# Attention scores turned on VectorE instead of TensorE, with a new start order and finer weight splits, in a fused attention, MLP and mixture-of-experts kernel

## What is computed

```python
scores  = scale * x @ state.T ;  a  = softmax(scores, -1) ;  xread = a @ state     # over Ns = 32
scores2 = scale * state @ x.T ;  a2 = softmax(scores2, -1);  sread = a2 @ x        # over S = 512
x = concat([xread, sread], 2) -> 4608 rows of 512
h = x @ w_in ; g = h * clip(h + 3, 0, 6) / 6 ; x = g @ w_out                       # first MLP
e_idx = argmax(x @ w_gate) ; out = gate * sigmoid(...) * (relu(x @ w1[e]) @ w2[e]) # one expert per row
```

## Time and profile before

| | us |
|---|---|
| median of 3 runs | 1210.06 (1208.73 to 1210.42) |
| the profiled execution | 1208.73 |
| its span, first to last instruction | 1207.0 |
| TensorE busy | 1170.7 (97%) |
| VectorE busy | 602.6 (50%) |
| ScalarE busy | 443.7 (37%) |

### The profile page before, as it was taken

One profiled execution on the slowest core, in us unless ns is written; L12 is line 12 of the kernel. 1 busy time (PEld: TensorE's weight loads), 2 busy tenths in 40 slices (PEclk: granted clock), 3 DMA queues, 4 the chain that ended last, 5 costly groups with the idle time before them and its releaser, 6 DMA issues.

```text
span 1207.0 us, 21126 instructions
## 1 busy us (share of the span) xinstructions
PE 1170.7 (97%) x6652; PEld 923.6 (77%) x6653; DVE 602.6 (50%) x1140; ACT 443.7 (37%) x741; POOL 83.9 (7%) x96
## 2 busy tenths in 40 slices
PE   8999999999999999999999987999999999999995
PEld 6777777777777777777778975888888888878874
DVE  5564644645536456455464355645453333666331
ACT  3454434443444344444544341423331112344110
POOL 0000100101001001010010110200000000000000
PEclk9999999999999999999999988999999999999998
DMA  9210110001101010010020365145151111442111
GB/s 368 71 36 1 71 36 36 36 36 71 35 1 71 36 35 36 36 71 1 1 105 1 122 226 171 54 175 188 33 189 37 52 35 45 179 152 59 46 37 42
DMA packets 46922, 91.45 MB, mean 76 GB/s; under 512 B 10751, under 2 KB 32895, under 8 KB 42496
## 3 DMA queue, kind: packets, MB, share of 16 engines
q1 hardware_dynamic: 41088, 72.57, 17.7%
q0 software_dynamic: 5760, 17.90, 3.9%
HBM read 65.95 MB, written 25.55 MB: 76 GB/s over the span
## 4 chain that ended last, share of the span: by engine, by line
PE 93%; DVE 3%; ACT 1%; issue 1%; DMA 0%; POOL 0%; DVEq 0%; ACTq 0%; SPq 0%; POOLq 0%
PE y_ps L840 31%; PE h_ps L896 17%; PE y_ps L922 17%; PE h_ps L825 14%; PE y_ps L908 3%; PE a_ps L800 2%; PE h_ps L815 2%; PE a_ps L690 1%; PE y_ps L861 1%; PE a_ps L778 1%; PE a_ps L751 1%; PE b_ps L698 1%; DVE we L469 1%; PE b_ps L690 1%; PE b_ps L715 0%
## 5 line engine op out<-in xcount | busy, mean ns | idle before, releaser
L840 PE MATMUL y_ps<-w_out_hi,hid_hi 128*128 128x512 f32 x544 | 220.4, 405 | 0.3 <-DVE w_out_lo L1329 0.3
L840 PE MATMUL y_ps<-w_out_hi,hid_lo 128*128 128x512 f32 x544 | 212.8, 391 | 0.0
L840 PE MATMUL y_ps<-w_out_lo,hid_hi 128*128 128x512 f32 x544 | 212.6, 391 | 0.0
L896 PE MATMUL h_ps<-we,xg_t_hi 128*128 (+1 forms) x608 | 197.4, 406 | 7.1 <-DVE xg_t_lo L1399 3.9
L922 PE MATMUL y_ps<-we,act_t_hi 128*128 (+1 forms) x608 | 187.9, 390 | 1.7 <-issue 1.7
L825 PE MATMUL h_ps<-att_hi,mix 128*128 128x512 f32 x512 | 185.6, 406 | 0.4 <-DVE att_lo L1212 0.4
L1344 DVE SCALAR_TENSOR_TENSOR hid<-hid,h_ps 128x512 f32<-128x512 f32 (+1 forms) x144 | 94.3, 655 | 181.8 <-ACT hid L1037 180.3
L1037 ACT ACTIVATE hid<-h_ps,three 128x512 f32<-128x512 f32 (+1 forms) x144 | 95.5, 663 | 203.1 <-PE h_ps L825 179.7
L840 PEld LDWEIGHTS y_ps<-w_out_hi,hid_hi 128*128 128x128 f32 x544 | 102.2, 188 | 51.2 <-issue 30.4
L896 PEld LDWEIGHTS h_ps<-we,xg_t_hi 128*128 128x128 f32 x608 | 113.6, 192 | 33.2 <-issue 8.4
L922 PEld LDWEIGHTS y_ps<-we,act_t_hi 128*128 128x128 f32 x608 | 114.1, 188 | 26.8 <-issue 2.0
(11 more groups left out here) (226 smaller groups left out, 1324.4 us busy)
## 6 DMA issues: line engine op xcount, KB each, us to landing
raw<-in_w SPq DMA_DIRECT2D x14, 2048.0 KB, 8.4
xg<-buckets SPq DMA_DIRECT2D x164, 64.0 KB
xb<-in_x_rows SPq DMA_DIRECT2D x8, 1024.0 KB, 4.8
x_t<-in_x_t SPq DMA_DIRECT2D x7, 1024.0 KB, 5.0
buckets<-pad_row SPq DMA_DIRECT2D x8, 774.0 KB, 8.7
w_in_raw<-in_w_in SPq DMA_DIRECT2D x4, 1024.0 KB, 13.1
raw_out<-in_w_out SPq DMA_DIRECT2D x4, 1024.0 KB, 14.7
x_t_second<-in_x_t SPq DMA_DIRECT2D x1, 1024.0 KB, 19.9
```

The costliest lines, as they stand in the source:

```text
L840: i = pe.matmul(y_ps[:, t, :], (hid_hi, hid_lo)[hp][:, hid_at(b, j), t * P:(t + 1) * P], w_out_s[wp][:, j, :], start=(j == 0 and m == 0), ...
L896: i = pe.matmul(hid_ps[:, h, :], xg_t[xp][:, slot % 2, k, :], we[:, bass.ds(w_at + (wp * WPART + k * F + h * BANK), BANK)], start=(k == 0 ...
```

## The change

- **Turning.** S1's banks are no longer copied. A step TURN on VectorE transposes each bank in 32 x 32 blocks straight into `sc1` (one instruction per group), which puts the 32 keys of a head along a row; MAX1, DIF1, EXP1 and NORM1 work there in place, NORM1 now group by group. A step BACK on VectorE transposes the weights back to `att1_raw` in SBUF, and A1's high and low parts are taken from that. S2 and A1 vanish from TensorE. SOFT2 reads the banks directly. `bank_free` after S1 now gives two conditions, the turn and the second softmax's exponential.
- **First two mixed steps.** M 0 and M 1 of block 0 both go to the banks of `y_ps` (0 and 1, 2 and 3) in the prologue; `mlp_second(0, 0)` waits before its third tile until both are read. M 2 of block 0 moves from half 20's table place to half 7 of `ATT_REST`.
- **Second weights.** Chunk 0's high part is made in one piece in the prologue. All low parts, and the high parts of chunks 1 to 3, are made step by step (128 x 512) at step j of block 0, and `mlp_second` waits for w_out_lo j + 1.
- **Order.** `ATT`, `ATT_FIRST`, `ATT_REST` are new; the loads at the start come in another order; `keep_warm` has 60, then 75, 55 and 30 after halves 0, 3 and 8, and 160 before the row stage.

```diff
-    ATT = {14: [("S1", 0)], 15: [("SOFT2", 0)], 16: [("SOFT2", 1), ("S2", 0), ("MAX1", 0)],
...
+    ATT = {14: [("S1", 0)], 15: [("TURN", 0), ("SOFT2", 0)], 16: [("TURN", 1), ("SOFT2", 1)],
...
-    SPLIT_OUT_FIRST = 6
-    SPLIT_OUT = {5: 1, 9: 2, 13: 3}
+    SPLIT_OUT_FIRST = 7
-    WARM_START, WARM, WARM_ROWS = 60, {2: 45, 5: 25, 11: 12}, 100
+    WARM_START, WARM, WARM_ROWS = 60, {0: 75, 3: 55, 8: 30}, 160
...
-        return y_ps[:, g, :] if a == 0 and f == 0 else bank_ap(g)
+        return y_ps[:, GROUPS * f + g, :] if a == 0 and f < 2 else bank_ap(g)
...
-                elif name == "S2":
-                    wait(pe, f"sc_t_ready{n}", a + 1)
-                    for c in range(CH):
-                        i = pe.transpose(bank_ap(k)[:, c * P:(c + 1) * P], scores_t(a)[:, n, c * P:(c + 1) * P],
-                                         ident[:])
...
-                elif name == "A1":
-                    wait(pe, "att1_ready", a + 1)
-                    for c in range(CH):
-                        i = pe.transpose(bank_ap(k)[:, c * P:(c + 1) * P], sc1[:, c, n * P:(n + 1) * P], ident[:])
...
-                pe.wait_ge(sem("w_out_lo"), j // GO + 1)
+                pe.wait_ge(sem("w_out_lo"), j + 1)
...
+                if is_b(b, 0) and j == 0 and t == 2:
+                    pe.wait_ge(sem("mix_ready"), GROUPS * 2)
...
-                    act.activation(scores_t(a)[:, 0, :], bank_ap(0), ACT.Copy).then_inc(sem("sc_t_ready0"), 1)
...
-                    dve.tensor_copy(scores_t(a)[:, 1, :], bank_ap(1)).then_inc(sem("sc_t_ready1"), 1)
...
+                elif name == "TURN":
+                    wait(dve, "s1_ps", a + 1)
+                    wait(dve, "att1_back", GROUPS * (a - 1) + n + 1)
+                    dve.transpose(sc1[:, n].rearrange("p k m -> p (k m)"), bank_ap(n)).then_inc(sem("sc1_turned"), 1)
...
+                elif name == "BACK":
+                    wait(dve, "h_ps", KF * a)
+                    wait(dve, "att1_ready", GROUPS * a + n + 1)
+                    dve.transpose(att1_raw[:, n, :], sc1[:, n].rearrange("p k m -> p (k m)")
+                                  ).then_inc(sem("att1_back"), 1)
...
-            js = slice(GO * c, GO * c + GO)
-            dve.tensor_tensor(w_out_s[LO][:, js, :], raw_out[:, js, :], w_out_s[HI][:, js, :].bitcast(F32),
+            dve.tensor_tensor(w_out_s[LO][:, j, :], raw_out[:, j, :], w_out_s[HI][:, j, :].bitcast(F32),
```

More of the change, by code:

```diff
@@ L332, in att_steps @@
         now = [(*step, 0) for step in ATT_REST.get(half, [])] if b == 0 else []
-        if b < B and half in MIX:
+        if b < B and half in (MIX_FIRST if b == 0 else MIX):
             now = now + [("M", MIX[half], b)]
@@ L683, in side @@
                 pb = b - 1
-                if (free := bank_free(b, half, k)) is not None:
+                for free in bank_free(b, half, k):
                     wait(pe, *free)
@@ L734, in side @@
                 k = BANK_OF.get((name, n))
-                if k is not None and (free := bank_free(b, half, k)) is not None:
+                for free in bank_free(b, half, k) if k is not None else ():
                     wait(pe, *free)
@@ L739, in side @@
                     for g in range(GROUPS):
-                        if (free := bank_free(b, half, g)) is not None:
+                        for free in bank_free(b, half, g):
                             wait(pe, *free)
@@ L785, in side @@
                     pe.transpose(bank_ap(k)[:, 0:P], sr_rows[:], ident[:]).then_inc(sem("srt_ps"), 1)
-                elif name == "A1":
-                    wait(pe, "att1_ready", a + 1)
-                    for c in range(CH):
-                        i = pe.transpose(bank_ap(k)[:, c * P:(c + 1) * P], sc1[:, c, n * P:(n + 1) * P], ident[:])
-                    i.then_inc(sem("a1_ps"), 1)
                 elif name == "M":
                     for g in range(GROUPS):
-                        if (name, n, a) != FIRST_MIX and (free := bank_free(b, half, g)) is not None:
+                        for free in bank_free(b, half, g) if (name, n, a) not in FIRST_MIX else ():
                             wait(pe, *free)
@@ L855, in mlp_block, with keep_warm @@
                     side(b, 2 * j + 1 if j < KF else KF + j)
-        def keep_warm(n):
+        def keep_warm(n, bank):
             for _ in range(n):
-                pe.matmul(y_ps[:, CH - 1, 0:P], ones[:], ones[:], start=True, stop=True)
+                pe.matmul(bank[:, 0:P], ones[:], ones[:], start=True, stop=True)
         pe.wait_ge(sem("ones_ready"), 1)
-        keep_warm(WARM_START)
+        keep_warm(WARM_START, h_ps[:, 1, :])
         for half in range(HALF):
@@ L867, in _ @@
             if half in WARM:
-                keep_warm(WARM[half])
+                keep_warm(WARM[half], h_ps[:, 1, :])
         for b in range(B):
@@ L1246, in side @@
[L1246 to L1248 removed]
+                    wait(dve, "exp1_ready", GROUPS * a + n + 1)
+                    dve.tensor_reduce(sum1[:, n], sc1[:, n], AX.X, ALU.add).then_inc(sem("sum1_ready"), 1)
+                    wait(dve, "sum1_ready", GROUPS * a + n + 1)
+                    dve.tensor_scalar(sum1[:, n], sum1[:, n], 1e-9, None, ALU.add).then_inc(sem("sum1_eps"), 1)
```

152 lines of the change are left out of this document (66 added, 86 removed), and 7 rows, old and new, of the table ATT.

## The result

| | before | after |
|---|---|---|
| median, us | 1210.24 (1208.73 to 1210.96, 4 runs) | 1192.26 (1189.99 to 1192.53, 4 runs) |
| profiled execution | 1208.73 | 1192.12 |
| its span | 1207.0 | 1190.4 |

The ratio is 0.9849, 95% interval 0.9832 to 0.9866: 18 us faster, against 17 forecast and a predicted time of 1193.0.

What follows compares the result with a forecast made beforehand. TensorE, busy 97% of the span, was taken as the bound. Savings of 6.5 us (prologue, block 0) and 10.5 us (later blocks) from 1208.73, plus 1.33 for the median, gave 1193.0 us; own range 1190 to 1196.

Steps and rivals of the forecast that it cites:

- Turning in the blocks: Blocks 1 to 6: 24 groups of four transposes leave TensorE at 0.44 us each, saving 10.5 us if VectorE keeps up.
- rival 5: A removed TensorE transpose is worth its whole length: 30.8 us instead of 12.3, time 1174.5; chance 0.01.
- Rivals 3 and 4: VectorE's order becomes the bound, slower than before, chance 0.03; removed TensorE time returns as bank waits, 1209 us, chance 0.02.
- The slack: Halves 15 to 18 of each block: tightest place, second(8) keeps 2.5 to 3 us; bank waits lie further out.
- Rival 3's bill: Seven blocks: slack of 2.75 us plus about 1.9 us VectorE free; gain eaten at a transpose of 3.5 us.
- Prologue and block 0: Start to block 1: block 1 begins at 97.6 instead of 104.14, 6.5 us earlier.
- The wait ahead of first(2): Block 0: first(2) could start at 22.45 but waits 0.2 us for step 0's product, ending 22.6.
- M 1: Second mixed step moves from block 0 to the prologue, under the wait for VectorE: 1.1 us saved.
- The split in pieces: Block 0: two TensorE waits, 0.64 and 1.43 us, go, saving 2.07; the pieces' VectorE cost is hidden.
- The prologue's fill: Fills in the prologue behind the first 60 cost 0.25 us at most, counted in the sum.
- The row stage: Row stage entry with 60 more fills: 0 entered, bounds -1.6 (all at full clock) to +3 (all at half).
- rival 2: Row stage: longer fill lengthens the pause before the second tile, its 24 matmuls run at half clock: +3, 1196; chance 0.07.

Runs made afterwards that it cites:

- control: The changed kernel run again with no edit, beside the kernel before: 1191.07 us, ratio 0.9847.
- the turning alone: The changed kernel with chunks, second mixed step, load order and 100 fills put back as before, new step tables kept: 1197.44 us, ratio 0.9906.
- the last two runs: The changed kernel with fills inside the row stage's first tile: 60 more there, 1187.51 us; 40 there with 100 before the stage, 1187.98 us.

## Why the prediction was right, and where it was not

**Turning in the blocks: right.** 10.5 us forecast, 10.58 found, and 593.4 in every kernel whose middle was left alone. The 96 added transposes returned 10.47, so rival 5 (the whole length of a removed transpose) is refuted from both sides. Rivals 3 and 4 fall with 0.72 us for a block transpose from PSUM.

**The slack: the step failed, the sum did not need it.** The prediction put the tightest place at second(8) with 2.5 to 3 us left, and said of the bank waits that they "lie further out still". Added work showed the reverse: in the middle TensorE stalled at A2 and M 3, both of which wait for a bank, and never at step 8, which took 5.2 us of delay with no wait but the 0.84 us or more at M 3 ahead of it. So step 8 had more room than counted, about 4.4 us. The slack is 1.9 us in the middle. I had counted the chain up to the hidden values' low part, but not the mix's low part and the exponential, which stand in the same engines' order and hold a bank until they are done. Rival 3's bill took 2.75 us of slack for its first term and would have fallen due earlier, with 1.9.

**Prologue and block 0: -6.5 forecast, -7.95 found.** 1.05 of the 1.45 between them is that the 60 fills ended earlier (5.33 against 6.38 us), which no edit causes. From the first step of block 0 at 18.54 (control) to block 1 it is 77.7 us, where the forecast has 76.6 behind the end of the first step at 21.05, thus 78.0 from its start at 19.65. The wait ahead of first(2) is there as the prediction has it, behind the product of step 0 that ends at 21.76 in the chain shown above. In the timeline it shows as a pair of matmuls over 1.00 us where the pair behind takes 0.63, so it is nearer to 0.4 us than to the 0.2 forecast:

```profile
21.30 1.00 PE L814 MATMUL h_ps<-att_hi,mix 128*128 128x512 f32 x2
```

**M 1: 1.1 forecast, 1.36 found.** Moving it adds waits of 0.26 and 0.40 us in block 0, takes the one ahead of first(2) away and lets the first step come 0.34 us sooner; the 1.36 is what is left.

**The split in pieces: the term was mis-stated.** The prediction booked 2.07 us for two old waits that go. Under the new step tables the chunks cost 9.9 us in block 0: 3.40 us of wait at second(8) where the old tables had 0.27, the lower clock behind it, and the two others. In the earlier trace rows the old kernel paid 2.07, and the 0.27 on top, which the prediction did not read. So the pieces do not add 2 us to what turning gives. They are what makes the new order of the block pay: the turning alone, with chunks, loses 1.7 us up to block 1 and keeps just the 10.6 of the middle. The sum came out because I counted the whole change against the old waits, not because I saw this.

**Load order: nothing, as forecast. The prologue's fill:** forecast to cost at most 0.25, it costs 0.3 and saves 1.3 behind it.

**The row stage: 0 forecast, +1.93 found; the weight of rival 2 was too low.** It had the right consequence (the longer fill lets the first tile end sooner, what follows idles longer and runs at half clock) and the wrong gap. The chain shows the 24 matmuls at 8.03 us against 7.24 in the earlier trace rows, 0.8 of the 1.93, and 7.5 to 8.7 in the other profiles with 160. The transposes ahead of them take 1.11 against 0.66 us, but cost nothing: the second tile starts 13.3 us behind the first with either. The largest part, 0.95, is that the first tile started later, and with 160 fills that start lies anywhere from 19.9 to 21.6 us behind the mark. In all nine profiles TensorE had ended its fills by then and waited for VectorE's low part of the rows, 0.3 to 1.8 us, so the fills do not hold it up; why it scatters is open. The gap's length alone does not explain the clock either: the turning alone, with 100 fills, had the same 3.44 us and its 24 matmuls took 7.40. With the gap filled they take 5.86. The row already told it: 7.24 against 5.61 was an opening of 1.6 us. The prediction saw the idle time and the lower level, gave "all at full clock" as a bound, and still entered 0.

So 1193.0 against 1192.26 is closer than the steps deserve, which is luck: 1.5 us gained early and 1.9 lost in the row stage cancel, and about 1 us of each lies in places that also scatter by as much between runs of other variants.

## What to carry to other kernels

Where an engine is busy all the time, price a removed instruction by its share of the chain of waits, not by its length: 0.11 us and not 0.27 here. Count slack to every buffer that in-order engines hand back, not only to the operand on the obvious path; add work in two sizes to find it. And when TensorE waits some microseconds in the middle of a kernel, look at the granted clock behind the wait: filling one such gap of 3.4 us brought 3.6 us in the medians, of which the trace assigns 2.5 to the matmuls behind it, while 60 more fills in front of the stage went with slower matmuls there.

## What the runs showed of the hardware that I had not expected

The same 60 matmuls of the first fill took from 4.82 to 6.38 us in fourteen profiles, and everything up to block 1 shifts by it.

How long TensorE was idle does not by itself tell what clock follows. Idle times of 3.40 and 3.44 us were followed by a granted clock of 0.50 to 0.51. The wait of 2.33 to 2.48 us that stands in each of blocks 1 to 6 with seven more block transposes left it at 1.00 four times, and was followed by 0.50 and 0.52 the other two, behind 2.48 and 2.46 us. In the profile of the result 1.83 us ahead of the first tile were followed by 0.61 from 711 to 713 us and 0.54 from 713 to 715; behind 2.27 us (the first wait with chunks) and the pauses of 1.2 us in the last two runs the matmuls kept their short times. And the kernel before was idle for 3.65 us in its prologue, with a granted clock of 1.00 from 14 to 24 us:

```profile
19.05 0.63 PE L790 MATMUL a_ps<-ident,sc 128*128 128x128 f32 x4 [3.65 <-DVE sc L1247]
...
710.45 0.71 PE L888 MATMUL h_ps<-we,xg_t_hi 128*128 128x512 f32 x2 [1.83 <-DVE xg_t_lo L1380]
```

(The first line is the kernel before, the second the result.) What decides it, no run here shows.

A block transpose of 128x512 fp32 on VectorE costs nearly what the copy of that size did in the kernel before (0.69 us), from either memory (0.72 and 0.71 us).
